# First two feed-forward chunks among the last attention pair's units, second product two chunks behind

## The reference

```
# 4 batches x 8 heads, 1152 keys, head size 64; pairs of queries are averaged: 576
q_pool = q.reshape(B, H, S // 2, 2, D).mean(axis=3)
scores = matmul(q_pool, k^T) / sqrt(D)
attn = exp(scores - max(scores)); attn = attn / (sum(attn) + 1e-09)
x = matmul(attn, v)  ->  2304 tokens x 512
h = x @ w_in;  g = h * sigmoid(h);  x = g @ w_out        # 512 -> 2048 -> 512
a = x @ w1;  b = x @ w2;  h = a * b @ w3;  out = h @ w_out2   # 512 -> 1024 -> 1024 -> 512
```

## Time and profile before

| what | value |
|---|---|
| three runs | 1279.23, 1280.03, 1280.61 us |
| profiled execution: time; span of its instructions | 1280.76 us; 1278.6 us |
| TensorE busy (matmuls) | 1268.6 us, 99% of the span |
| VectorE, ScalarE, GpSimd busy | 601.3, 587.6, 378.1 us |
| last pair's first scores; its last values end; first full-array matmul | 510.98; 541.1; 541.18 us |
| mean of VectorE's pL, of its gL; ScalarE's first-tile weight copy | 0.75, 0.64; 0.62 us |
| third slice of w_out: issued; landed after | 543.78; 2.8 us |

### The profile page before, as it was taken

The page is one execution under the profiler, slowest core; times in us unless marked ns, Lnnn a source line. Parts: engine busy times, 40 slices in busy tenths (PEclk is TensorE's granted clock), DMA queues, the critical chain, the costliest instruction groups (busy, mean ns, idle before and its releaser), DMA issues.

```text
span 1278.6 us, 26209 instructions
## 1 busy us (share of the span) xinstructions
PE 1268.6 (99%) x10968; PEld 1148.6 (90%) x10968; DVE 601.3 (47%) x895; ACT 587.6 (46%) x1065; POOL 378.1 (30%) x321
## 2 busy tenths in 40 slices
PE   8999999999999999999999999999999999999998
PEld 7999999999999999888888888888988888888888
DVE  6778877777787778723212121111155222222222
ACT  3777777777777777833222222222245212121111
POOL 5577777777777776210000000000000000000000
PEclk9999999999999999999999999999999999999999
DMA  4222222222222211021000000001062000000001
GB/s 143 66 75 73 66 73 72 74 76 75 75 75 75 75 57 38 27 68 50 9 1 1 1 1 1 1 1 50 1 207 74 1 26 8 10 24 1 33 8 42
DMA packets 26005, 58.59 MB, mean 46 GB/s; under 512 B 7200, under 2 KB 8736, under 8 KB 25888
## 3 DMA queue, kind: packets, MB, share of 16 engines
q1 hardware_dynamic: 25888, 56.91, 13.4%
HBM read 52.04 MB, written 4.79 MB: 44 GB/s over the span
## 4 chain that ended last, share of the span: by engine, by line
PE 97%; DVE 2%; DMA 0%; ACT 0%; issue 0%; DVEq 0%; ACTq 0%
PE psum L957 19%; PE psum L958 19%; PE psum L959 19%; PE psum L1035 18%; PE psum L974 10%; PE psum L1010 9%; PE psum L1012 3%; DVE mx L745 1%; PE psum L985 1%; DMA qraw<-in_qT 0%; DVE pL L780 0%; ACT pH L566 0%; PE psum L1045 0%; ACT tmpB L559 0%; ACT pF L574 0%
## 5 line engine op out<-in xcount | busy, mean ns | idle before, releaser
L745 DVE TENSOR_REDUCE mx<-psum 128x2 f32<-128x768 f32 x240 | 229.0, 958 | 85.3 <-PE psum L974 82.1
L566 ACT ACTIVATE pH<-psum 128x576 fp32r<-128x576 f32 x288 | 188.5, 655 | 133.9 <-PE psum L1012 129.1
L471 POOL TENSOR_TENSOR pL<-pF,pH 128x576 fp32r<-128x576 f32 x120 | 170.2, 1428 | 111.6 <-ACT pF L574 111.4
L888 DVE TENSOR_TENSOR gL<-gF,gH 128x512 fp32r<-128x512 f32 (+1 forms) x80 | 51.1, 639 | 310.2 <-ACT gH L647 310.2
L1035 PE MATMUL psum<-pH,vH 64*128 64x288 f32 x1152 | 180.5, 295 | 0.9 <-ACT tmpB L559 0.5
L1035 PE MATMUL psum<-pL,vH 64*128 64x288 f32 x1152 | 178.6, 292 | 0.8 <-DVE pL L780 0.8
L1035 PE MATMUL psum<-pH,vL 64*128 64x288 f32 x1152 | 178.5, 292 | 0.0
L644 ACT ACTIVATE gF<-psum 128x512 f32<-128x512 f32 (+1 forms) x80 | 44.4, 555 | 269.9 <-PE psum L959 269.9
L935 DVE TENSOR_TENSOR pr<-aS,psum 128x512 f32<-128x512 f32 (+1 forms) x40 | 25.4, 635 | 200.2 <-ACT aS L716 200.2
L1035 PEld LDWEIGHTS psum<-pH,vH 64*128 64x128 f32 x1152 | 117.0, 185 | 2.4 <-PE psum L1035 1.6
L957 PE MATMUL psum<-gH,woH 128*128 128x512 f32 (+1 forms) x320 | 117.9, 368 | 0.0
(11 more groups left out here) (104 smaller groups left out, 2762.5 us busy)
## 6 DMA issues: line engine op xcount, KB each, us to landing
vraw<-in_v SPq DMA_DIRECT2D x16, 576.0 KB, 4.5
qraw<-in_qT SPq DMA_DIRECT2D x15, 576.0 KB, 5.5
kraw<-in_kT SPq DMA_DIRECT2D x15, 576.0 KB, 3.7
rsums<-recips SPq DMA_DIRECT2D x32, 144.0 KB, 3.0
wstage<-in_w_in SPq DMA_DIRECT2D x16, 256.0 KB, 4.1
fstage<-in_w3T SPq DMA_DIRECT2D x8, 512.0 KB, 4.4
w12stage<-in_w SPq DMA_DIRECT2D x8, 512.0 KB, 4.7
outT<-oS SPq DMA_DIRECT2D x4, 1024.0 KB, 4.2
```

What stands on the lines that cost most here:

```text
L471: pool.tensor_tensor(pL[r][:], pF[SLOT[n]][:], pH[r][:].bitcast(F32), ALU.subtract).then_inc(pL_pool, 1)
L566: act.activation(pH[r][:], scores, ACT.Exp, scale=SCALE).then_inc(pH_ready, 1)
L745: dve.tensor_reduce(mx[:, qt, :, kb], bank[:, :, 0:KW], AX.X, ALU.max).then_inc(max_taken, 1)
L888: dve.tensor_tensor(gL[r][:, w], gF[:, w], gH[r][:, w].bitcast(F32), ALU.subtract).then_inc(gL_ready, 1)
```

## The change

1. `early_slot`, `early`: the first products of chunks 0 and 1 of tile 0 (24 matmuls) are issued during the last pair, one or two at a time: after `score_t` in most units (after the values in units 0 and 9), by the table `EARLY_AT`, and twice among the last values.
2. `x_hi_first`, `x_lo_first`: tile 0's split moves to the pair before the last, its low part from VectorE to GpSimd.
3. GpSimd's `normalize` of pair 14 waits until all low parts pL are done; `take_o` of the last pair comes after chunk 0's low part on VectorE, its reciprocals after chunk 2's.
4. `second1` runs two chunks behind `first1` in place of one.
5. Buffers lie elsewhere, so that what is used earlier is free earlier; ScalarE's waits for the end of attention move from chunk 0 to chunk 1.

```diff
@@ -315,6 +316,11 @@
 
         def own(j):
             return slice(D * j, D * j + D)
+
+        EARLY = 2 * 3 * KC
+        EARLY_AT = {0: 1, 2: 2, 3: 2, 4: 2, 5: 2, 6: 2, 7: 1, 8: 1, 9: 1, 11: 2, 12: 1, 13: 1, 14: 1, 15: 1, 16: 1, 17: 1}
+        EARLY_END = 2
+        assert sum(EARLY_AT.values()) + EARLY_END == EARLY
...
@@ -476,6 +482,11 @@
                 cols = slice(i * WSLICE, (i + 1) * WSLICE)
                 pool.tensor_tensor(winL[:, cols], wstage[:], winH[:, cols].bitcast(F32), ALU.subtract
                                    ).then_inc(winL_ready, 1)
+
+            def x_lo_first(k):
+                pool.wait_ge(xH_ready, k + 1)
+                pool.tensor_tensor(xL[1][:, k, width(0)], xT[:, k, span(0)], xH[1][:, k, width(0)].bitcast(F32),
+                                   ALU.subtract).then_inc(xL_ready, 1)
...
+                else:
+                    x_lo_first(0)
...
-                    normalize(p - 1, 1, (qL_ready, 2 * (p + 2) + 1) if more2 else (winL_ready, p + 1))
+                    normalize(p - 1, 1, (qL_ready, 2 * (p + 2) + 1) if more2 else (xL_ready, 2))
...
             w_lo(p)
+            pool.wait_ge(pL_dve, LO_DVE)
             normalize(p - 1, 1, (winL_ready, PAIRS))
             normalize(p - 1, 0, (normalized, 2 * p - 1))
             normalize(PAIRS - 1, 1, (normalized, 2 * p))
...
+            def x_hi_first(k):
+                act.wait_ge(normalized, 2 * HPB)
+                act.copy(xH[1][:, k, width(0)], xT[:, k, span(0)]).then_inc(xH_ready, 1)
...
+                    if p == PAIRS - 2 and u in (5, 8, 11, 14):
+                        x_hi_first((u - 5) // 3)
...
-            act.wait_ge(vL_ready, KB * PAIRS)
-            act.wait_ge(normalized, 2 * (PAIRS - 1))
-            x_hi(0, 1, xH_ready, (h_ready, 0))
...
+                    if first and c == 1:
+                        act.wait_ge(vL_ready, KB * PAIRS)
+                        act.wait_ge(pL_dve, LO_DVE)
+                        act.wait_ge(pL_pool, LO_POOL)
+                        act.wait_ge(winL_ready, PAIRS)
+                        act.wait_ge(pv_done, 2 * ALL)
...
-            x_lo(0, 1, xH_ready, xL_ready)
-            take_o(PAIRS - 1, 1)
...
                     if c == 0 and first:
+                        take_o(PAIRS - 1, 1)
+                    if c == 2 and first:
                         guard_sums(PAIRS - 1)
                         recip(PAIRS - 1)
...
+            def early_slot(i):
+
+                c, k, s = i // (3 * KC), i // 3 % KC, i % 3
+                if i == 0:
+                    pe.wait_ge(winH_ready, (KC - 1) * FF // WSLICE + 1)
+                    pe.wait_ge(winL_ready, (KC - 1) * FF // WSLICE + 1)
+                if c == 0 and s == 0:
+                    pe.wait_ge(xL_ready, k + 1)
+                weights, x = ((winH, xH[1]), (winH, xL[1]), (winL, xH[1]))[s]
+                last = pe.matmul(hbank[c][:, width(0)], weights[:, k * FF + c * P:k * FF + (c + 1) * P],
+                                 x[:, k, width(0)], start=(k == 0 and s == 0), stop=(k == KC - 1 and s == 2))
+                if k == KC - 1 and s == 2:
+                    last.then_inc(h_ready, 1)
+
+            def early(first, count):
+
+                for i in range(first, first + count):
+                    early_slot(i)
+                return first + count
...
+                    if u % NC != 0:
+                        done = early(done, ahead)
...
+                    if u % NC == 0:
+                        done = early(done, ahead)
+            done = early(done, 1)
             values(ALL - 3, 1)
             values(ALL - 2, 0)
+            done = early(done, 1)
             values(ALL - 2, 1)
             values(ALL - 1, 0)
             values(ALL - 1, 1)
...
-            def tile1(t, e):
-
-                first = isinstance(t, int) and t == 0
-                for c in range(C1):
-                    first1(t, e, c)
-                    if c > 0:
-                        second1(t, c - 1, first)
-                    elif not first:
-                        second1(t - 1, C1 - 1, isinstance(t, int) and t == 1)
-
-            for t in range(TILES):
-                tile1(t, (t + 1) % 2)
+            for n in range(2, TILES * C1):
+                first1(n // C1, (n // C1 + 1) % 2, n % C1)
+                second1((n - 2) // C1, (n - 2) % C1, n - 2 < C1)
+            second1(TILES - 1, C1 - 2)
             second1(TILES - 1, C1 - 1)
```

More of the change, by code:

```diff
@@ L100, in block_kernel @@
         hold.enter_context(nc.sbuf_tensor("held_for_weights", [P, 2 * KC * FF], F32))
+        ffn = ExitStack()
+        xH, xL = [None, sb("xH1", [KC, TILE], F32R, ffn)], [None, sb("xL1", [KC, TILE], F32R, ffn)]
         with ExitStack() as st:
             tmpA[0], tmpB[0] = sb("tmpA0", [2, HALF], F32, st), sb("tmpB0", [2, HALF], F32, st)
+            pF = [sb(f"pF{r}", [2, HALF], F32, st) for r in range(2)]
+            vL = sb("vL", [NC, 3, D], F32R, st)
             kraw = sb("kraw", [S], F32, st)
@@ L106, in block_kernel @@
             qsum = sb("qsum", [Q], F32, st)
[L107 to L112, removed]
+            kH, kL, qH, qL, mrow = ([None, None] for _ in range(5))
+            for j in range(2):
+                if j == 1:
+                    vraw = sb("vraw", [NC, P], F32, st)
+                kH[j] = sb(f"kH{j}", [S], F32R, st)
+                kL[j] = sb(f"kL{j}", [S], F32R, st)
+                qH[j] = sb(f"qH{j}", [QPAD], F32R, st)
+                qL[j] = sb(f"qL{j}", [QPAD], F32R, st)
+                mrow[j] = sb(f"mrow{j}", [QPAD], F32R, st)
             vH = sb("vH", [NC, 3, D], F32R, st)
-            vL = sb("vL", [NC, 3, D], F32R, st)
-            pF = [sb(f"pF{r}", [2, HALF], F32, st) for r in range(2)]
             pH = [sb(f"pH{r}", [2, HALF], F32R, st) for r in range(RING)]
@@ L123, in block_kernel @@
             selR = sb("selR", [P], F32R, st)
[L125 to L132, removed]
         with ExitStack() as st:
-            woH = sb("woH", [C1, DM], F32R, st)
-            woL = sb("woL", [C1, DM], F32R, st)
-            wostage = [wstage, sb("wostage1", [DM], F32, st)]
+            fstage = [sb(f"fstage{r}", [FOLDW], F32, st) for r in range(2)]
+        xH[0], xL[0] = sb("xH0", [KC, TILE], F32R, ffn), sb("xL0", [KC, TILE], F32R, ffn)
+        with ExitStack() as st:
             gF = sb("gF", [TILE], F32, st)
@@ L139, in block_kernel @@
             gL = [sb(f"gL{r}", [TILE], F32R, st) for r in range(2)]
+            wo = sb("wo", [C1, 2, DM], F32R, st)
+            woH, woL = wo[:, :, 0, :], wo[:, :, 1, :]
+            wostage = [wstage, sb("wostage1", [DM], F32, st)]
         foldH = sb("foldH", [C2, DM], F32R, ffn)
@@ L249, in block_kernel @@
         FP = FOLDW // DM
-        FOLD_UNDER = -(-(2 * C2 * DM + 3 * FOLDW - C1 * DM) // DM)
+        FOLD_UNDER = -(-(2 * C2 * DM + 3 * FOLDW - 5 * TILE) // (2 * DM))
         LAG = 2
@@ L527, in _ @@
                     q_lo(p + 2, 0)
+                else:
+                    x_lo_first(1)
                 if not first:
-                    normalize(p - 1, 1, (qL_ready, 2 * (p + 2) + 1) if more2 else (winL_ready, p + 1))
+                    normalize(p - 1, 1, (qL_ready, 2 * (p + 2) + 1) if more2 else (xL_ready, 2))
                 p_lo(n + 10)
@@ L535, in _ @@
                     k_lo(p + 2, 0)
+                else:
+                    x_lo_first(2)
                 p_lo(n + 15)
@@ L540, in _ @@
                     k_lo(p + 2, 1)
+                else:
+                    x_lo_first(3)
             p = PAIRS - 1
@@ L652, in take_y @@
                     act.copy(xT[:, m, span(t)], accbank[m][:, width(t)]).then_inc(y_taken, 1)
[L654 to L657, removed]
             def fold_hi(c):
@@ L1055, in _ @@
             keep_busy(8)
+            done = 0
             for p in range(PAIRS):
@@ L1060, in _ @@
                     item = item_at(p, u)
+                    ahead = EARLY_AT.get(u, 0) if p == PAIRS - 1 else 0
                     if u % NC == 1 and n > LAG:
```

## The result

The changed kernel takes 1282.89 us, median of 13 runs (1282.54 to 1283.65), against 1280.03 us for before (13 runs): ratio 1.0025, interval 1.0018 to 1.0032. It is slower by 2.9 us, and the forecast was 3.3.

A forecast was written before the change was run, and what follows sets the result against it. TensorE, with 97% of the chain at full clock, was taken to bound the kernel. Waits gone (-3.9), 18 x 0.40 us of shape changes (+7.2) and 0 elsewhere gave +3.3 us: 1283.3 us, range 1278.3 to 1286.6.

The forecast's parts named there:

- Where the time is lost, and what can be won: TensorE in the last pair: waits in eight places, covered by early products or gone, gain 3.9 us.
- the stretch: From the last pair's first scores to the first full-array matmul of the feed-forward stage; forecast 39.0 us, before 30.2.
- 18 entries at 0.20: Last pair, TensorE: each change from half-array to full-array matmuls costs 0.20 us, bounds 0 and 0.38.
- 18 exits at 0.20: Last pair, TensorE: each change from full-array back to half-array matmuls costs 0.20 us, bounds 0 and 0.38.
- The sum: Whole kernel: -3.9 for waits, +7.2 for shape changes, 0 for the rest, together +3.3 us.
- Rival A: Last pair: only half-to-full changes cost, 3.6 against 3.9 us; -0.3, 1279.7 us, no change; chance 0.20.
- rival B: Last pair: shape changes cost nothing, all 3.9 us gained; 1276.1 us, 0.3% faster; chance 0.12.
- Rival C's chain: Feed-forward start: w_out's fourth slice, loaded behind the reciprocals' spreading, 1.5 us late; main forecast 0; rival 1285 to 1287, chance 0.18.

The follow-up runs named there:

- without early matmuls: Changed kernel with all 24 early products computed after the last values, rest of the change kept; 1277.95 us, 0.9989 of before.
- half-array steps placed by the waits: Against before: the change with early products as 64-row steps, two or four at measured waits, SP's reciprocal spreading moved ahead of w_out's sixth slice; 1276.24 us, 0.9975.
- two groups: Changed kernel with the 24 early matmuls in two groups of 12, in units 2 and 11, instead of 18 groups; 1278.53 us, 0.9994 of before.
- half-array steps: Changed kernel with the same 24 products as 64-row steps of 512 columns into two PSUM banks, in 16 groups; 1277.90 us, 0.9989 of before.
- 24 groups: Changed kernel with its 24 early matmuls in 24 groups of one instead of 18 groups of one or two; 1285.19 us, 1.0046 of before.
- a second kernel: Changed kernel with early products after the last values and GpSimd's pair 14 normalization back beside VectorE's low parts; 1279.00 us, 0.9996 of before.

## Why the prediction was right

**Where the time is lost, and what can be won.** Right: 3.93 us of waits in eight places went, 1.31 of them by the normalization (shown without early matmuls), the rest by cover (shown with half-array steps placed by the waits, where the stretch is 3.5 us shorter and VectorE's late addition costs 0.2 at its end). The prediction names 0.38 for a wait; those of units 2 and 11 were 0.58 and 0.56, with one more late step each, which the 3.9, taken from all starts, held already. Counting starts, not busy time, was what made this visible.

**18 entries at 0.20.** Right: 0.10 and 0.11 in each, in every group. The one entry in before had been a fair sample.

**18 exits at 0.20, which no row had shown.** Right, and in part by luck: 0.09 to 0.10 and 0.10 to 0.11. The price was carried over from the nearest row, a single entry, to something that no row showed and that could have cost anything from 0 to 0.38. Half the price is the late first start, the other half the late start of the one behind it, as behind a wait. "TensorEngine Tiling (Array Packing)" of the Trainium skill, section Key Properties, says that changing the tiling mode drains TensorE. The trace agrees in so far as both directions cost the same 0.20 us.

**The sum.** +3.3 forecast, +3.4 in the stretch, +3.3 from F to the end, +2.9 between the medians, where 0.34 us outside the span counts against it. Neither term hid an error of the other: the waits gave 3.9 and the changes took 7.2 to 7.3.

**Rival A** (exits free, 35.4 us for the stretch) and **rival B** (changes free, 31.8) fall with 39.06; that the price hangs on the number of groups is shown by 2, 18 and 24 of them. "TensorE: Matmul & The Clock Gate" of the Trainium skill, Part 2, has LDWEIGHTS pulled ahead of matmuls in flight. The trace shows that within one shape and not across a change: the first weight load behind an entry has 0.16 us idle before it, behind an exit 0.24 or more, and both start with their own matmul.

**Rival C's chain.** It was counted at 0 with nothing to spare, from before's own intervals put together in a new order, so that it held was partly luck. In the changed kernel the load was issued at 560.18, 11.4 us after the values ended (forecast 11.5), and landed after 3.5 us. ScalarE waited 7.2 us for it and TensorE not at all:

```profile
563.73 0.62 ACT L695 CAST wo<-wostage 128x512 fp32r<-128x512 f32 x1 [7.21 <-DMA wostage<-in_w_out]
564.26 0.59 ACT L667 ACTIVATE gF<-psum 128x512 f32<-128x512 f32 x1
...
565.38 0.39 PE L980 MATMUL psum<-xH,winH 128*128 128x512 f32 x1
```

The silu ended half a microsecond ahead of chunk 5's first product. With two groups and with half-array steps it was 0.8 and 1.1 us late, so it hid there some of what they won.

**What was a little off.** VectorE's low parts took 0.76 us nearly throughout; single ones were longer (1.12 at 528.09, beside GpSimd's work on w_in). Chunk 0's low part gL took 1.74 us at 548.33, beside the delayed normalization at 548.09. Neither was waited for.

## What to carry to other kernels

A busy TensorE can hide its own stalls: measure from start to start, and look at the weight loads' idle time marked "issue". Work used to fill a wait has to have the shape of its neighbours: here a change of shape and back cost 0.40 us, as much as the waits that it was to fill. The same products split over 64 rows and two banks cost nothing extra on TensorE, and with better places and SP's load moved they turned +2.9 us into -3.6. A filler should cover the wait and the late weights behind it (0.25 + 0.11): one step of 0.228 us left the 0.11, two left nothing. And a chain with half a microsecond to spare must be counted again when the part ahead of it changes.

## What the runs showed of the hardware

- A change between 64-row (288 columns) and 128-row (512 columns) matmuls costs 0.20 us in either direction, and 0.395 us per group by the stretch of 24 groups against 18. A change from 288 to 512 columns at 64 rows costs nothing.
- Profiled executions of these closely related programs differ in the distance of TensorE's first maxima (0.32 or 0.18 us between the same steps), and reach the last pair up to 1.1 us sooner or later, though the granted clock reads 1.00 in the window of 6 to 8 us in both. That one program does both is not shown; its two bunches of times suggest it.
- Behind a matmul that came 3.0 us late the clock was at 1.2 GHz (0.50 in the window of 543.0 to 546.2), with nine starts up to 0.20 late: a second cost of about 1.6 us beside the wait itself.
- Four of VectorE's subtractions of 128 x 576 took 5.27 us beside GpSimd's multiplications (4.91 in a second kernel), and 0.76 us each without them.
